# An attention and MLP kernel on one core: less work for first tiles, a split first load, moved weight pieces, and a reordered drain

## The chip, the cores and the metric

The kernel runs on one core of a Trainium2 chip. The metric is the device time of the program in microseconds (us), lower is better. The kernel before took 481.90, 483.58 and 482.17 us in three runs; the median is 482.17.

The engines of a core: TensorE (PE, matrix products, with its weight loads listed apart as PEld), VectorE (DVE), ScalarE (ACT), GpSimd (POOL), and SyncE (SP), which here only issues transfers (DMA). Each works through its own list of instructions; they wait for each other by semaphores.

## The reference

Three layers in a row, in 32-bit floats: an attention with a distance bias and a mask, an MLP mixer, and a gated MLP with a spatial mix. Only the first and the start of the second matter here.

```python
# q, k, v: batch 2, heads 8, seq 768, head_dim 64; n_global = 8, n_local = 96
scores = (q @ k.T) / sqrt(D)
rel = pos[:, None] - pos[None, :]
is_global = pos[None, :] < n_global
is_local = (rel >= 0) & (rel < n_local)
keep = is_global | is_local
dist = where(is_global & ~is_local, n_local, abs(rel))
scores = where(keep, scores - slope[h] * dist, -1e9)
a = softmax(scores)
x = a @ v                          # heads side by side: (2, 768, 512)
h = relu(x.T @ w_tok1) @ w_tok2    # token mix, over the 768 tokens
u = x + h.T
x2 = u + relu(u @ w_ch1) @ w_ch2
# then: u, v = relu(x2 @ w_in) in halves; layer norm of v; spatial mix; gate; w_out
```

## The kernel before

**Tiles.** The 768 positions are six tiles of 128. A query tile needs the keys of its own tile, the last 96 of the tile before, and the first 32 (the global ones). So the host lays out, for each head pair and tile, two blocks of 128 keys: the tile's own, and the tile before with the 32 global keys written over its first columns. For tile 0 the two blocks are: the 32 global keys with zeros behind, and the tile's own. The values are laid out alike. Whether `n_global` and `n_local` fit this form is computed on the device (`flag`); if not, a general path runs (`Else` branches), which is not used with these inputs.

**Pairs and batches.** Two heads (64 rows each) make a pair, 2 x 4 = 8 pairs (`PAIRS`). A batch is two tiles of one pair, so 24 batches (`BATCHES`), three per pair (`PER_PAIR`). q, k and v of a pair lie in one of two buffers. Batches 0, 3, 6, ..., 21 hold tile 0.

**A batch.** `scores(j)`, line 1074: for each tile and head, PE multiplies 128 queries by 256 keys, into PSUM. DVE reads the result with the bias added and takes the maximum (line 830), ACT takes the exponent (line 600), PE transposes the four blocks per tile (`transpose_probs`, line 1063), ACT (line 607, first tile) and DVE (line 838, second tile) copy them out, PE multiplies by the values (`values`, line 1101), ACT copies the product (`oT`, line 612), PE turns it back (`turn_o`, line 1063), DVE divides by the sum into `X32` (line 854), and POOL splits that into a high and a low part `Xh`, `Xl` (`split_batch`, lines 523 and 525). Each code matmul in 32-bit floats appears as two instructions in the trace, a transpose as one.

**The order** is written out by hand on each engine. A round j of PE is: transposes of batch j+1, scores of j+3, values of j, turn of j-1. DVE and ACT have orders of their own, two batches apart.

**Before the first scores** DVE builds `dist` (128 x 384: 128 columns for tile 0's first block, 128 for the own tile, 128 for the tile before) from `rel`, waits for `n_words` (the two counts, 16 bytes per partition, first in SP's queue), and multiplies it by the slopes of heads 0 and 1 (line 817); POOL makes the tables of heads 2 to 7 (line 515). Tile 0 reads columns 0 to 255, other tiles 128 to 383. SP loads q of pair 0, v of 0, q, k, v of 1, ten weight pieces of 256 KB, and then, as buffers come free, `load_qk(n)` after the scores of pair n-2 and `load_v(n)` after its values. ACT issues k of pair 0 (line 593).

**Weight pieces.** A piece lands in a staging slot and is split into a high part (copy) and a low part (subtraction), since later products multiply in three terms, high x high, high x low, low x high (`three`, lines 392 to 394). The first ten (`EARLY_END`: six for the token mix, four for `wc2`) are split by POOL before its first `split_batch` (lines 382 and 387).

**After the attention** PE computes four token products (`x.T @ w_tok1`, 18 matmuls of 512 columns each, two per image), ACT and DVE take the results in two parts (`A1`, line 648) after `attention_done`, which DVE signals when all of `X32` is written. Product 0 and 1 need the first image's x, 2 and 3 the second's (`x_lo`).

Of the kernel before, what the change touches and what calls it, by code (L numbers as in the profile page):

```python
# [21 lines left out]
def build(nc, n_both, qp, kp, vp, w_tok1, w_tok2, w_ch1, w_ch2, w_in, w_spatial, b_spatial, w_out, out):  # L22
# [25 lines left out]
    with ctx:  # L48
# [94 lines left out]
        loc = scratch("loc", [P, 2 * P], F32)  # L143
        tmp = scratch("tmp", [P, 2 * P], F32)
        causal = scratch("causal", [P, 2 * P], F32)
        loc0 = scratch("loc0", [P, GK], F32)
# [35 lines left out]
        flag_ready = sem("flag_ready")  # L182
        ident_ready = sem("ident_ready")
        dist_ready = sem("dist_ready")
        bias_ready = sem("bias_ready")
        pe_passed = sem("pe_passed")
        qk_landed = [sem("qk_landed0"), sem("qk_landed1")]
# [111 lines left out]
        EARLY_END = TOK_END + EARLY  # L299
        C2_END = len(pieces)  # L300
# [127 lines left out]
        def _(sp):  # L428
# [10 lines left out]
            sp.dma_start(qT[:, 0, :], qp[0, 0, :, :]).then_inc(qk_landed[0], 16)  # L439
# [14 lines left out]
            with sp.Else():  # L454
                with sp.Fori(0, B) as b:
                    with sp.Fori(0, HP) as hp:
                        for h in range(2):
                            with sp.Fori(0, NT) as t:
# [5 lines left out]
                                for first, t0, t1 in ((P, 0, 1), (0, 1, NT)):  # L464
# [3 lines left out]
                                for blk, t0, t1 in ((1, 0, 1), (0, 1, NT)):  # L468
# [21 lines left out]
        def _(pool):  # L490
# [40 lines left out]
            def first_pieces():  # L531

                for s in range(EARLY_END):
                    split_hi(pool, s)
                    split_lo(pool, s)
            with pool.If(fast):
                first_pieces()
                for j in range(BATCHES):
                    pool.wait_ge(x_written, j + 1)
                    split_batch(j)  # L540
            with pool.Else():
# [6 lines left out]
                first_pieces()  # L548
# [43 lines left out]
        def _(act):  # L592
            act.dma_start(kk[:, 0, :, :], kp[0, 0, :, :, :]).then_inc(qk_landed[0], 16)

            def exps(j, i):
                if i == 0:
                    wait(act, den_ready, 2 * (j - SUMS) + 1)
                for h in range(2):
                    act.wait_ge(scores_read, 4 * j + 2 * i + h + 1)
                    act.activation(prob[:, j % 3, i, h, :], prob[:, j % 3, i, h, :], ACT.Exp,  # L600
# [3 lines left out]
            def copy_probs(j):  # L604
                act.wait_ge(pt_ready, 2 * j + 1)
                wait(act, o_ready, j - 1)
                act.activation(probT[:, j % 2, 0, :], ps[:, PT, :], ACT.Copy).then_inc(pt_copied_act, 1)
# [37 lines left out]
            for n in range(B * TB):  # L645
                b, tb = divmod(n, TB)
                act.wait_ge(a1_ready, n + 1)
                act.activation(A1[0][:, b, tb, :], ps[:, n, :], ACT.Relu).then_inc(a1_hi, 1)
# [128 lines left out]
        def _(dve):  # L777
            done = [0]

            def step(*instructions):  # L780

                done[0] += len(instructions)
                for ins in instructions:
                    ins.then_inc(dve_setup, 1)
                dve.wait_ge(dve_setup, done[0])

            dve.wait_ge(pool_setup, 3)
            step(dve.tensor_copy(rel[:, :], rel_i[:, :]),
                 dve.tensor_copy(col[:, :], col_i[:, :]),
                 dve.memset(dist[:, GK:P], MASKED))  # L790
            step(dve.tensor_scalar(causal[:, :], rel[:, :], 0.0, None, ALU.is_ge))
# [12 lines left out]
            step(dve.scalar_tensor_tensor(out=loc[:, :], in0=rel[:, :], scalar=nl, in1=causal[:, :],  # L804
                                          op0=ALU.is_lt, op1=ALU.mult),
                 dve.tensor_scalar(glob[:, :], col[:, :], ng, None, ALU.is_lt))
            step(dve.scalar_tensor_tensor(out=loc0[:, :], in0=loc[:, 0:GK], scalar=0.0, in1=glob[:, :],
                                          op0=ALU.is_le, op1=ALU.mult),
                 dve.tensor_scalar(tmp[:, :], loc[:, :], -MASKED, MASKED, ALU.mult, ALU.add),
                 dve.tensor_scalar(glob[:, :], glob[:, :], -MASKED, MASKED, ALU.mult, ALU.add))  # L810
            step(dve.tensor_scalar(loc0[:, :], loc0[:, :], -MASKED, MASKED, ALU.mult, ALU.add),
                 dve.tensor_tensor(dist[:, P:2 * P], rel[:, 0:P], tmp[:, 0:P], ALU.max),
                 dve.tensor_tensor(dist[:, 2 * P + GK:3 * P], rel[:, P + GK:2 * P], tmp[:, P + GK:2 * P], ALU.max),
                 dve.tensor_scalar(dist[:, 2 * P:2 * P + GK], glob[:, :], nl, None, ALU.max))
            step(dve.tensor_scalar(dist[:, 0:GK], loc0[:, :], nl, None, ALU.max))
            dve.sem_inc(dist_ready, 1)
            step(*[dve.tensor_scalar(bias[:, h, :], dist[:, :], -(2.0 ** (-8.0 * (h + 1) / H)) / SCALE, None, ALU.mult)
                   for h in range(2)])

            def scores(j, i):  # L820
# [5 lines left out]
                if t == 0 and b == 0 and hp > 0 and i == 0:  # L826
                    dve.wait_ge(bias_ready, 2 * hp)
                at = 0 if t + i == 0 else P
                for h in range(2):
                    dve.tensor_tensor_reduce(prob[:, j % 3, i, h, :],  # L830
                                             ps[:, SC + 2 * (j % 2) + h, i * 2 * P:(i + 1) * 2 * P],
                                             bias[:, 2 * hp + h, at:at + 2 * P], -SCALE, 3.0e38, ALU.add, ALU.min,
# [26 lines left out]
            scores(0, 0)  # L859
            scores(0, 1)  # L860
# [200 lines left out]
        def _(pe):  # L1061
# [3 lines left out]
            def scores(j):  # L1065

                n, buf, t, b, hp = place(j)
                if t == 0:
# [266 lines left out]
```

## Time and profile before

| | |
|---|---|
| three runs | 481.90, 482.17, 483.58 us |
| profiled execution, its own time | 483.63 us |
| its span (first to last instruction) | 481.8 us |
| PE busy | 469.0 us, 97% |
| DVE, ACT, POOL busy | 187.4, 160.3, 130.2 us |
| DMA moved | 33.10 MB, mean 69 GB/s |

The span is one execution recorded by the hardware profiler; 1.8 us of the time lie outside it. The page gives busy time per engine, the span in forty slices, and the chain that ended last: followed back from the last instruction, at each step to what released it or to the instruction before it on its engine. The other views list instructions in order of time, or sum them over stretches. Matmuls overlap one another, so that a merged piece of several is shorter than their durations summed.

### The profile page before, as it was taken

How to read it: one execution, taken by the hardware profiler on the slowest of the kernel's cores; microseconds unless marked ns; L12 is line 12 of the kernel's file. 1: busy time of each engine (PE TensorE's matmuls, PEld its weight loads, DVE VectorE, ACT ScalarE, POOL GpSimd, SP SyncE). 2: the span in 40 equal slices, each digit the busy share in tenths (PEclk: the TensorE clock that was granted, in tenths of full speed). 3: DMA queues.
4: the chain of work that ended last, by engine and by line, in shares of the span. 5: the costliest groups of instructions: out<-in, count | busy, mean ns of one | idle time of the engine just before them, and what ended most of it. 6: DMA issues, size and time to landing. Idle time of an engine off the chain costs nothing.

```text
span 481.8 us, 7048 instructions
## 1 busy us (share of the span) xinstructions
PE 469.0 (97%) x2664; PEld 400.3 (83%) x2664; DVE 187.4 (39%) x519; ACT 160.3 (33%) x415; POOL 130.2 (27%) x145
## 2 busy tenths in 40 slices
PE   4999999999999999999999999999989999999997
PEld 3777778789988888888888888888879898899985
DVE  5888999426432111511113311104773054204230
ACT  3888888327410000210011211213432213411211
POOL 5996332424232222310002222231670002400000
PEclk9999999999999999999999999999989999999999
DMA  8956545024411121000000011021000100100002
GB/s 323 321 205 236 216 167 199 3 67 152 132 65 45 44 51 60 0 1 0 1 0 0 2 33 34 0 87 35 0 1 0 54 13 1 44 23 1 1 37 94
DMA packets 13618, 33.10 MB, mean 69 GB/s; under 512 B 1552, under 2 KB 3088, under 8 KB 13584
## 3 DMA queue, kind: packets, MB, share of 16 engines
q1 hardware_dynamic: 13440, 31.86, 19.0%
q10 hardware_dynamic: 144, 0.79, 0.4%
q8 instruction: 21, 0.34, 0.3%
q14 instruction: 13, 0.11, 0.1%
HBM read 29.49 MB, written 3.15 MB: 68 GB/s over the span
## 4 chain that ended last, share of the span: by engine, by line
PE 93%; DVE 3%; ACT 1%; DMA 1%; issue 1%; SPq 0%; DVEq 0%
PE ps L392 25%; PE ps L394 25%; PE ps L393 25%; PE ps L1063 6%; PE ps L1074 5%; PE ps L1101 5%; PE ps L1162 1%; DMA qT<-in_q_pairs 1%; DVE V L1021 1%; DVE stats L1012 1%; ACT V L688 1%; DVE xsum L985 0%; DVE wo_h L382 0%; ACT Vn_h L703 0%; DVE xsum L988 0%
## 5 line engine op out<-in xcount | busy, mean ns | idle before, releaser
L997 DVE SCALAR_TENSOR_TENSOR R_l<-ps,R_h 128x512 fp32r<-128x512 f32 x36 | 24.9, 692 | 134.9 <-ACT R_h L674 134.9
L674 ACT ACTIVATE R_h<-ps 128x512 fp32r<-128x512 f32 x36 | 21.4, 595 | 130.5 <-PE ps L394 130.5
L394 PE MATMUL ps<-UT_h,wc_l 128*128 128x512 f32 x144 | 56.0, 389 | 0.0
L393 PE MATMUL ps<-UT_l,wc_h 128*128 128x512 f32 x144 | 56.0, 389 | 0.0
L392 PE MATMUL ps<-UT_h,wc_h 128*128 128x512 f32 x144 | 56.0, 389 | 0.0
L600 ACT ACTIVATE prob<-prob,neg_max 128x256 f32<-128x256 f32 x96 | 47.5, 498 | 7.3 <-DVE neg_max L830 7.3
L567 POOL TENSOR_TENSOR UT_l<-xsum,UT_h 128x512 fp32r<-128x512 f32 x12 | 16.3, 1365 | 84.3 <-ACT UT_h L665 84.3
L392 PE MATMUL ps<-R_h,wc2a 128*128 128x512 f32 x96 | 37.3, 389 | 0.0
L393 PE MATMUL ps<-R_l,wc2a 128*128 128x512 f32 x96 | 37.3, 389 | 0.0
L394 PE MATMUL ps<-R_h,wc2a 128*128 128x512 f32 x96 | 37.3, 389 | 0.0
L830 DVE CUSTOM_DVE_ANT_0 prob<-ps,bias 128x256 f32<-128x256 f32 x96 | 35.6, 412 | 0.7 <-PE ps L1074 0.7
L1074 PE MATMUL ps<-kk,qT 64*128 64x256 f32 x192 | 28.8, 423 | 6.4 <-DMA qT<-in_q_pairs 6.4
L392 PE MATMUL ps<-wsp_h,Vn_h 128*128 128x384 f32 x96 | 32.8, 342 | 2.2 <-DVE xsum L985 2.2
L393 PE MATMUL ps<-wsp_l,Vn_h 128*128 128x384 f32 x96 | 32.8, 342 | 0.0
L394 PE MATMUL ps<-wsp_h,Vn_l 128*128 128x384 f32 x96 | 32.7, 341 | 0.0
L394 PEld LDWEIGHTS ps<-UT_h,wc_l 128*128 128x128 f32 x144 | 27.1, 188 | 5.7
L393 PEld LDWEIGHTS ps<-UT_l,wc_h 128*128 128x128 f32 x144 | 27.0, 188 | 5.6
L392 PEld LDWEIGHTS ps<-UT_h,wc_h 128*128 128x128 f32 x144 | 27.0, 188 | 5.5
L573 POOL TENSOR_TENSOR Vn_l<-V,Vn_h 128x512 fp32r<-128x512 f32 x12 | 16.3, 1362 | 56.0 <-ACT Vn_h L703 56.0
L1035 DVE TENSOR_TENSOR gate<-ps,b_all 128x384 f32<-128x384 f32 x16 | 8.9, 558 | 54.9 <-PE ps L394 54.9
L1074 PEld LDWEIGHTS ps<-kk,qT 64*128 64x128 f32 x192 | 17.7, 198 | 11.8 <-DMA qT<-in_q_pairs 6.4
L1101 PEld LDWEIGHTS ps<-probT,vv 128*64 128x64 f32 x384 | 20.5, 136 | 7.6 <-issue 7.3
(132 smaller groups left out, 1013.8 us busy)
## 6 DMA issues: line engine op xcount, KB each, us to landing
vv<-in_v_pairs SPq DMA_DIRECT2D x8, 768.0 KB, 4.5
kk<-in_k_pairs SPq DMA_DIRECT2D x7, 768.0 KB, 7.3
staged<-in_moe_w_ch SPq DMA_DIRECT2D x20, 256.0 KB, 2.7
qT<-in_q_pairs SPq DMA_DIRECT2D x8, 384.0 KB, 5.2
out<-out_sb SPq DMA_DIRECT2D x12, 256.0 KB, 2.0
staged<-in_moe_w_spatial SPq DMA_DIRECT2D x9, 256.0 KB, 2.6
staged<-in_moe_w_in SPq DMA_DIRECT2D x8, 256.0 KB, 2.6
staged<-in_moe_w_tok SPq DMA_DIRECT2D x6, 256.0 KB, 9.8
```

What stands on the lines that cost most here:

```text
L392: pe.matmul(o, a[0], b[0], start=start, stop=False, skip_group_check=True)
L393: pe.matmul(o, a[0], b[1], start=False, stop=False, skip_group_check=True)
L394: return pe.matmul(o, a[1], b[0], start=False, stop=stop, skip_group_check=True)
L567: pool.tensor_tensor(u, xsum[:, i % 2, :], UT[0][:, d, c * CH:(c + 1) * CH].bitcast(F32), ALU.subtract).then_inc(x2_lo, 1)
L573: pool.tensor_tensor(Vn[1][:, t, :], V32[:, n % 3, :], Vn[0][:, t, :].bitcast(F32), ALU.subtract).then_inc(vn_lo, 1)
L600: act.activation(prob[:, j % 3, i, h, :], prob[:, j % 3, i, h, :], ACT.Exp, bias=neg_max[:, j % 3, i, h:h + 1], scale=-1.0, accum_out=sums ...
L674: act.activation(R[0][:, f % 3, :], ps[:, 4 + f % 4, :], ACT.Relu).then_inc(ring_hi, 1)
L830: dve.tensor_tensor_reduce(prob[:, j % 3, i, h, :], ps[:, SC + 2 * (j % 2) + h, i * 2 * P:(i + 1) * 2 * P], bias[:, 2 * hp + h, at:at + 2 ...
L997: dve.scalar_tensor_tensor(out=R[1][:, f % 3, :], in0=ps[:, 4 + f % 4, :], scalar=0.0, in1=R[0][:, f % 3, :].bitcast(F32), op0=ALU.max, op ...
L1063: return pe.transpose(o, x, ident[:, :])
L1074: last = pe.matmul(ps[:, SC + 2 * (j % 2) + h, i * 2 * P:(i + 1) * 2 * P], qT[rows, buf, (t + i) * P:(t + i + 1) * P], kk[rows, buf, t + i ...
L1101: last = pe.matmul(ps[Dh * h:Dh * (h + 1), OB, o:o + P], vv[:, buf, t + i, blk, h, :], probT[:, j % 2, i, (2 * h + blk) * P:(2 * h + blk + ...
```

## The change

1. *Merged table for first tiles.* Tile 0 uses one key block, its own tile, with a table that takes for the first 32 columns the smaller of the local and the global distance. Its scores, transposes, copies and values are one block wide instead of two (`blocks(j, i)`); other tiles keep two. The host layout follows. DVE's table code has a new order: the 128 columns of tile 0 and their two heads first, the rest (`other_tiles`) after the first reads.
2. *First q, k transfer in two.* The columns for batch 0 come first, counted by `qk_first`; `scores(0)` waits for them, `scores(1)` for the rest.
3. *Weight pieces behind later pairs.* SP issues two pieces after each `load_v(n)`, n = 2 to 6, instead of all ten at the start; POOL splits each between batches.
4. *Tile of ones on PE.* DVE first fills `oT` with ones; PE multiplies it by itself twice (512 columns) into a bank not yet in use, before `scores(0)`.
5. *Token product in the drain.* `token_hidden(0)` is issued before the last turn instead of after it.

The core of the diff:

```diff
+            first = BATCH * P
+            sp.dma_start(qT[:, 0, 0:first], qp[0, 0, :, 0:first]).then_inc(qk_first, 16)
+            sp.dma_start(qT[:, 0, first:S], qp[0, 0, :, first:S]).then_inc(qk_landed[0], 16)
             load_v(0)
             load_qk(1)
             load_v(1)
-            for s in range(EARLY_END):
-                load_piece(sp, s)
...
                     load_qk(n)
                     sp.wait_ge(o_ready, PER_PAIR * (n - 1))
                     load_v(n)
+                    for s in range(2 * (n - 2), min(2 * (n - 1), EARLY_END)):
+                        load_piece(sp, s)
...
+            piece_after = {PER_PAIR * (s // 2) + 2 + s % 2: s for s in range(EARLY_END)}
             with pool.If(fast):
-                first_pieces()
                 for j in range(BATCHES):
                     pool.wait_ge(x_written, j + 1)
                     split_batch(j)
+                    if j in piece_after:
+                        split_piece(piece_after[j])
...
-            act.dma_start(kk[:, 0, :, :], kp[0, 0, :, :, :]).then_inc(qk_landed[0], 16)
+            act.dma_start(kk[:, 0, 0:BATCH, :], kp[0, 0, :, 0:BATCH, :]).then_inc(qk_first, 16)
+            act.dma_start(kk[:, 0, BATCH:NT, :], kp[0, 0, :, BATCH:NT, :]).then_inc(qk_landed[0], 16)
...
+            dve.memset(oT[:, :, :], 1.0).then_inc(ones_ready, 1)
             dve.wait_ge(pool_setup, 3)
...
+            step(dve.tensor_scalar(late[:, 0:P], rel[:, 0:P], nl, MASKED, ALU.is_ge, ALU.mult),
+                 dve.tensor_scalar(glob[:, :], col[:, :], ng, MASKED, ALU.is_ge, ALU.mult))
+            step(dve.tensor_tensor(dist[:, 0:P], rel[:, 0:P], late[:, 0:P], ALU.max),
+                 dve.tensor_scalar(glob[:, :], glob[:, :], nl, None, ALU.max))
+            step(dve.tensor_tensor(dist[:, 0:GK], dist[:, 0:GK], glob[:, :], ALU.min))
+            step(*first_heads(slice(0, P)))
+            step(dve.tensor_scalar(late[:, P + GK:2 * P], rel[:, P + GK:2 * P], nl, MASKED, ALU.is_ge, ALU.mult),
+                 dve.tensor_tensor(dist[:, P:2 * P], rel[:, 0:P], late[:, 0:P], ALU.max),
+                 dve.tensor_copy(dist[:, 2 * P:2 * P + GK], glob[:, :]))
+            def other_tiles():
+                step(dve.tensor_tensor(dist[:, 2 * P + GK:3 * P], rel[:, P + GK:2 * P], late[:, P + GK:2 * P], ALU.max))
+                dve.sem_inc(dist_ready, 1)
+                step(*first_heads(slice(P, 3 * P)))
...
             scores(0, 0)
+            other_tiles()
             scores(0, 1)
...
+        def blocks(j, i):
+            return 1 if j % PER_PAIR == 0 and i == 0 else 2
...
-                        last = pe.matmul(ps[:, SC + 2 * (j % 2) + h, i * 2 * P:(i + 1) * 2 * P],
+                        wide = blocks(j, i) * P
+                        last = pe.matmul(ps[:, SC + 2 * (j % 2) + h, i * 2 * P:i * 2 * P + wide],
                                          qT[rows, buf, (t + i) * P:(t + i + 1) * P],
-                                         kk[rows, buf, t + i, :], start=True, stop=True)
+                                         kk[rows, buf, t + i, 0:wide], start=True, stop=True)
...
+            pe.wait_ge(ones_ready, 1)
+            for _ in range(2):
+                pe.matmul(ps[:, XB, :], oT[:, 0, 0:P], oT[:, :, :].rearrange("p a b -> p (a b)"), start=True, stop=True)
             scores(0)
             scores(1)
...
+                token_hidden(0)
                 turn_o(BATCHES - 1)
...
-            for n in range(B * TB):
+            for n in range(1, B * TB):
+                token_hidden(n)
```

Transposes, copies, exponents and values take `blocks(j, i)` in the same way. `token_hidden(n)` is the body of the former loop.

## Rows read from the trace of the kernel before

**Rows 1.** The page, busy time: engine, us, share of the span, instructions.
```profile
PE 469.0 (97%) x2664; PEld 400.3 (83%) x2664; DVE 187.4 (39%) x519; ACT 160.3 (33%) x415; POOL 130.2 (27%) x145
```

**Rows 2.** The chain in order of time: start us, us, what.
```profile
6.44 3.79 PE ps L1074 x16
10.23 1.98 PE ps L1063 x8
...
14.88 1.06 PE ps L1074 x8
...
84.61 1.02 PE ps L1101 x16
```

**Rows 3.** Timeline of PE, a steady round: start us, us, instruction, count.
```profile
50.27 1.04 PE L1063 MATMUL ps<-ident,prob 128*128 128x128 f32 x8
51.23 1.14 PE L1074 MATMUL ps<-kk,qT 64*128 64x256 f32 x8
52.30 1.09 PE L1101 MATMUL ps<-probT,vv 128*64 128x128 f32 x16
53.32 0.44 PE L1063 MATMUL ps<-ident,oT 128*128 128x128 f32 x2
```

**Rows 4.** Timelines of PE, pieces cut by a window's edge.
```profile
23.84 0.82 PE L1063 MATMUL ps<-ident,prob 128*128 128x128 f32 x6
...
54.56 0.70 PE L1074 MATMUL ps<-kk,qT 64*128 64x256 f32 x4
...
82.76 0.61 PE L1101 MATMUL ps<-probT,vv 128*64 128x128 f32 x8
```

**Rows 5.** Windows, PEld: stretch, us, busy (instructions), clock, DMA share, GB/s.
```profile
51.33:51.44 0.11, 0.11 (x4) 1.00 0.00 0
```

**Rows 6.** Windows, one round: busy of PE, PEld, DVE, ACT, POOL.
```profile
50.27:53.60 3.33, 3.33 (x37) 2.61 (x36) 3.06 (x12) 2.82 (x11) 1.13 (x2) 1.00 0.00 0
```

**Rows 7.** Timeline, the same round, DVE after its wait; idle before in brackets.
```profile
50.53 0.42 DVE L854 TENSOR_TENSOR X<-ps,recip 128x256 f32<-128x256 f32 x1 [0.27 <-PE ps L1063]
```

**Rows 8.** Timeline of the start: DVE to the first read, and a POOL split.
```profile
5.02 0.17 DVE L796 CAST n_lo<-n_words 128x2 f32<-128x2 uint32 x1 [2.67 <-DMA n_words<-in_n_both]
...
5.62 0.48 DVE L804 SCALAR_TENSOR_TENSOR loc<-rel,n_val,causal 128x256 f32<-128x256 f32 x1 [0.17 <-DVE n_val L798]
...
7.93 0.94 DVE L817 TENSOR_SCALAR bias<-dist 128x384 f32<-128x384 f32 x2
8.90 0.42 DVE L830 CUSTOM_DVE_ANT_0 prob<-ps,bias 128x256 f32<-128x256 f32 x1
...
16.09 1.28 POOL L387 TENSOR_TENSOR wt_l<-staged,wt_h 128x512 fp32r<-128x512 f32 x1 [0.15 <-POOL wt_h L382]
```

**Rows 9.** DMA queues from 3.0 to 3.75 us (q10 ACT's, q1 SP's).
```profile
DMA packets 94, 0.29 MB, mean 386 GB/s; under 512 B 47, under 2 KB 47, under 8 KB 94
...
q10 hardware_dynamic: 47, 0.29, 92.4%
```

**Rows 10.** DMA issues from 53 to 56 us, and the windows after them.
```profile
kk<-in_k_pairs SPq DMA_DIRECT2D x1, 768.0 KB, 7.3
...
54.40:59.40 5.00, 5.00 (x53) 3.75 (x52) 4.73 (x18) 4.49 (x16) 2.20 (x4) 1.00 0.98 354
```

**Rows 11.** Timeline of the attention's end.
```profile
89.41 0.44 PE L1063 MATMUL ps<-ident,oT 128*128 128x128 f32 x2
...
90.53 0.41 PE L1063 MATMUL ps<-ident,oT 128*128 128x128 f32 x2 [0.68 <-DVE X L854]
...
90.91 0.47 PE L392 MATMUL ps<-Xh,wt_h 128*128 128x512 f32 x1
...
95.34 0.60 ACT L648 ACTIVATE A_h<-ps 128x512 fp32r<-128x512 f32 x1 [5.43 <-PE ps L394]
```

**Rows 12.** Timeline and windows near 353 us: PE after its idle, clock 0.50.
```profile
352.85 0.41 PE L392 MATMUL ps<-wsp_h,Vn_h 128*128 128x384 f32 x1 [2.19 <-DVE xsum L985]
...
353.60:356.90 3.30, 3.30 (x13) 3.30 (x12) 1.73 (x3) 1.64 (x3) 3.30 (x3) 0.50 0.02 5
```

More of the change, by code:

```diff
@@ L453, in _ @@
                     load_v(n)
+                    for s in range(2 * (n - 2), min(2 * (n - 1), EARLY_END)):
+                        load_piece(sp, s)
             with sp.Else():
+                for s in range(EARLY_END):
+                    load_piece(sp, s)
                 with sp.Fori(0, B) as b:
@@ L529, in _, with split_piece @@
             fast = pool.value_load(flag[0:1, 0:1], min_val=0, max_val=1)
[L531 to L535, printed above, removed]
+            def split_piece(s):
+                split_hi(pool, s)
+                split_lo(pool, s)
+            piece_after = {PER_PAIR * (s // 2) + 2 + s % 2: s for s in range(EARLY_END)}
             with pool.If(fast):
[L537 removed]
                 for j in range(BATCHES):
@@ L547, in _ @@
                 pool.iota(a_col_i[:, :], pattern=[[1, S]], base=0, channel_multiplier=0).then_inc(pool_setup, 1)
-                first_pieces()
+                for s in range(EARLY_END):
+                    split_piece(s)
                 pool.wait_ge(a_x, UNITS * 2 + 1)
@@ L785, in step @@
                 dve.wait_ge(dve_setup, done[0])
+            dve.memset(oT[:, :, :], 1.0).then_inc(ones_ready, 1)
             dve.wait_ge(pool_setup, 3)
             step(dve.tensor_copy(rel[:, :], rel_i[:, :]),
-                 dve.tensor_copy(col[:, :], col_i[:, :]),
-                 dve.memset(dist[:, GK:P], MASKED))
-            step(dve.tensor_scalar(causal[:, :], rel[:, :], 0.0, None, ALU.is_ge))
+                 dve.tensor_copy(col[:, :], col_i[:, :]))
+            step(dve.tensor_scalar(late[:, :], rel[:, :], 0.0, MASKED, ALU.is_lt, ALU.mult))
+            step(dve.tensor_tensor(rel[:, :], rel[:, :], late[:, :], ALU.max))
             dve.wait_ge(n_landed, 16)
@@ L811, in _ @@
[L811 to L816, printed above, removed]
@@ new lines, in _, with first_heads @@
+            step(dve.tensor_tensor(dist[:, 0:GK], dist[:, 0:GK], glob[:, :], ALU.min))
+            def first_heads(columns):
+                return [dve.tensor_scalar(bias[:, h, columns], dist[:, columns], -(2.0 ** (-8.0 * (h + 1) / H)) / SCALE,
+                                          None, ALU.mult) for h in range(2)]
+            step(*first_heads(slice(0, P)))
+            step(dve.tensor_scalar(late[:, P + GK:2 * P], rel[:, P + GK:2 * P], nl, MASKED, ALU.is_ge, ALU.mult),
+                 dve.tensor_tensor(dist[:, P:2 * P], rel[:, 0:P], late[:, 0:P], ALU.max),
+                 dve.tensor_copy(dist[:, 2 * P:2 * P + GK], glob[:, :]))
@@ L1112, in turn_o, with token_hidden @@
                 last.then_inc(xb_ready, 1)
+            pe.wait_ge(ones_ready, 1)
+            for _ in range(2):
+                pe.matmul(ps[:, XB, :], oT[:, 0, 0:P], oT[:, :, :].rearrange("p a b -> p (a b)"), start=True, stop=True)
             scores(0)
             scores(1)
+            def token_hidden(n):
+                b, tb = divmod(n, TB)
+                if n == 0:
+                    wait_pieces(pe, 0, TOK_END)
+                if tb == 0:
+                    pe.wait_ge(x_lo, BATCHES // B * (b + 1))
+                for t in range(NT):
+                    last = three(pe, ps[:, n, :], [w[:, t, tb * P:(tb + 1) * P] for w in wt1],
+                                 [x[:, b * NT + t, :] for x in (Xh, Xl)], t == 0, t == NT - 1)
+                last.then_inc(a1_ready, 1)
             pe.wait_ge(ident_ready, 1)
@@ L1144, in _ @@
                     last.then_inc(a_o, 1)
-            wait_pieces(pe, 0, TOK_END)
-            for n in range(B * TB):
-                b, tb = divmod(n, TB)
-                if tb == 0:
-                    pe.wait_ge(x_lo, BATCHES // B * (b + 1))
-                for t in range(NT):
-                    last = three(pe, ps[:, n, :], [w[:, t, tb * P:(tb + 1) * P] for w in wt1],
-                                 [x[:, b * NT + t, :] for x in (Xh, Xl)], t == 0, t == NT - 1)
-                last.then_inc(a1_ready, 1)
+                token_hidden(0)
+            for n in range(1, B * TB):
+                token_hidden(n)
             for n in range(B * DB * 2):
```

58 lines of the change are left out of this document (27 added, 31 removed).

## The prediction

> **What bounds the kernel now.** I read the page first: TensorE (PE) is busy 97% of the span [rows 1]. The edits lie in the first 91 us, so the chain in order of time comes next [rows 2]. Until 6.44 us PE waits for the first q and k. From there to 14.88 us the chain hops between PE, VectorE (DVE) and ScalarE (ACT): a ramp. From 14.88 to 84.61 us PE alone is on it. The timeline of PE shows a round of that stretch: eight transposes, eight score matmuls, sixteen value matmuls, two turns, from 50.27 to 53.60, no idle time on a row [rows 3]. In that round DVE is busy 3.06 us of 3.33 and ACT 2.82 [rows 6]; DVE would be the next bound. The end of the attention shows a PE wait before the last turn [rows 11]. Ahead of the attention DVE builds the bias table [rows 8].
>
> I sum against the profiled execution's own time, 483.63 us (span 481.8, 1.8 around it). The timed runs were 481.90, 482.17 and 483.58, so the profiled one is like the slowest. Its extra 1.5 us has a visible source: for 3.3 us from 353.6 the granted clock is 0.50, that is 1.2 GHz of 2.4, after PE had idled 2.19 us [rows 12]. Half of 3.3 us is 1.65. I take it that the median run lacks this.
>
> **One key block for first tiles.** Batches that begin with tile 0 (8 of 24, one per head pair) use one block there.
> Transposes: 2 of 8 go. A piece with six lasts 0.82 us, one with eight 1.04 [rows 3, 4]: 0.11 each, so 0.22.
> Values: 4 of 16 go. The two heads run as a pair; x8 against x16 is 0.61 against 1.09 us [rows 3, 4], 0.12 a pair of instructions. I take 0.11, as for a transpose, which also streams 128 columns: 0.22.
> Scores: 4 of 8 instructions shrink from 256 to 128 columns. x4 against x8 is 0.70 against 1.14, 0.21 to 0.22 per pair of heads [rows 3, 4]. If a narrow pair costs the 0.11 of 128 columns, two save 0.21. Bounds: 0, if loading 128 columns of weights for each head is the limit, and 0.21. I take 0.21, because between 51.33 and 51.44 four weight loads of this line were under way [rows 5]: the heads load side by side, a pair per 0.11 us.
> The Trainium skill (TensorE: Matmul & The Clock Gate, LDWEIGHTS) says that a load takes its columns, 107 ns for 128, whatever the rows. Taken one after the other, a narrow pair would stay at 0.21 and the sum would be 1.5 us smaller; taken side by side it agrees with the row.
> The steady stretch holds scores and transposes of seven pairs (pair 0's are in the ramp) and values of eight: 7 x 0.22 + 8 x 0.22 + 7 x 0.21 = **4.8 us**. Is it all on the path? Three rounds fall from 9.99 to 9.34 us on PE. DVE needs 3 x 3.06 = 9.18, less two reads shortened from 256 to 128 columns (0.42 us each now [rows 8], some 0.13 less): 8.9. ACT needs 8.5 less narrower work. PE stays the bound by 0.4 us in three rounds. The shortest PE round is 3.33 - 0.43 = 2.90, 0.16 below DVE's 3.06, and DVE is early by 0.27 us a round, which it spends waiting for PE's turn [rows 7].
>
> **The start.** Four edits, one question: when are the first scores read, now at 8.90 [rows 8], and what follows?
> DVE's path. It takes up n_words at 5.02, starts the first wide operation 0.60 later and reads 3.28 after that [rows 8]. New order before the first read: compares of 128 and 32 columns, then max of each, 0.45 a step; min of 32, 0.25; two heads of 128, 0.45 (two of 384 took 0.94); then compare of 160, max of 128, copy of 32, 0.7. Together 2.3 us: DVE saves 1.0.
> n_words. 16 bytes per partition, yet DVE idled 2.67 us for it [rows 8]. In 0.75 us both queues moved 47 packets: every small one takes turns with a 6 KB one of k [rows 9]. The first k transfer now has 2 KB packets, a third of the time: 47 packets in 0.75 us on 16 engines are 0.25 us each, so the five to six turns still ahead of each engine at 3.0 us shrink from 1.4 us to 0.5. Bounds for the gain 0 and 1.0; I take 1.0, as the turns are seen one to one.
> The Trainium skill (DMA: Bandwidth & Descriptors, Queues, rings and completion order) lets an engine drain some 9 to 17 descriptors of one queue before it turns to the other. Then k's packet size would hardly matter to n_words and the gain would be 1.0 us smaller. The row disagrees.
> So DVE could read at 8.90 - 2.0 = 6.9.
> PE's path. The first scores need 128 KB of q and 256 KB of k. Q comes behind n_words and alternates with the rest of k, so 0.9 of the former 1.15 MB pass first; at the 386 GB/s of [rows 9] 0.7 us sooner, 5.75 instead of 6.44. Sixteen score instructions took 3.79 us [rows 2], 0.47 a pair; this batch has two wide and two narrow pairs, 1.4 us and 0.2 for the last to end: 7.4. At twice the clock it is 6.6.
> The product of ones is four instructions of 512 columns, 0.85 us each by that slow pace (0.43 to 0.47 for 256), from about 1.5 us, behind a memset on DVE, which waits for POOL then anyway, to 5.0. It ends before q arrives. Before, transposes at 10.23 took 1.98 us for eight [rows 2] against 1.04 later [rows 3]: the slow level lasted until about 12. From 1.5 on, the same 6 us would raise the clock about the first scores. If the ones do nothing for the clock, S(0) and S(1) still end by 9.3, before their readers come to S(1).
> First read between 6.9 and 7.9; I take 7.2, 1.7 sooner.
> After it. The other tiles' table (a max, two heads of 256 columns: 1.0 us) now stands before the second pair of reads. From first read to the steady scores at 14.88 it took 6.0 us. Add 1.0, less 0.3 for two narrow reads, less 0.5 for transposes at full clock: 6.2. Steady scores start at 13.4: **1.5 us**, bounds 0.6 and 2.1. POOL's tables for the other heads start, as now, near 8 and are needed two at a time from batch 3 on.
>
> **Weight pieces later.** Ten pieces of 256 KB leave the start, where nothing waited for them: 0. Now two follow the v of pairs 2 to 6 on SP's queue, ahead of the next pair's q and k. K issued at 54.27 landed 7.3 us later, at 61.6; 512 KB more at 354 GB/s add 1.5, and two more issues lie under the transfer: 63.1. That pair's scores are due at 64.56, 63.9 with shorter rounds [rows 10]. Cover 0.8 us; cost 0. POOL splits a piece in 1.28 us and a cast [rows 8], beside 1.13 of its own per round [rows 6]: it fits, and no one waits for it before 83 us.
>
> **Token product in the drain.** Turn 22 starts at 89.41, turn 23 at 90.53 after 0.68 us idle, token matmuls at 90.91 [rows 11]. With 18 token matmuls before turn 23 the idle time goes: **0.7 us**; bounds 0.5 and 0.8. They need the first image's x alone. Later by some 4 us come the last x, attention_done and POOL's split of it; they are wanted by product 2, a whole product after turn 23 (product 0 started at 90.91 and ACT took its result at 95.34 [rows 11]), and take some 2. ACT's first copy waits for attention_done about as long as for its product now.
>
> **Sum.** 4.8 + 1.5 + 0.7 = 7.0 us: 483.63 becomes 476.6 with the slow stretch, 482.17 becomes **475.2** for the median.
>
> **Rivals.**
> A, narrow scores save nothing (weights loaded one after the other), 1.5 back: 476.7. For it: both heads load as many columns as before; against it [rows 5]. Chance 0.17.
> B, the slow clock stretch is in the median run: two of four executions have the longer time, and the edits shift the work. The Trainium skill (the same TensorE page, HAM oscillation) has the clock fall after idle PE. From [rows 12]: plus 1.6, 476.8. Chance 0.17.
> C, n_words lands as before and the ones do nothing: first read 7.9, gain of the start 0.8, 475.9. Chance 0.1.
> D, slower: pieces hold up q and k. It decides once k lands over 0.8 us behind my 63.1. At half the rate (3 us for two pieces) and with both issues unhidden (0.7) it lands at 65.3, 1.4 us late; five pairs cost 7.0 and eat the gain, and a little slower still ends at 483 to 484. Against: the rate in the row. Chance 0.03.
> E, no change to speak of: a chain through DVE, not PE, paces the rounds at 3.33; only start and drain remain, 480.0. Against: DVE's wait in [rows 7]. Chance 0.05.
> The forecast has 0.48. The range goes down by the start's upper bound (0.6), the drain's (0.1) and as much again for what neither bound holds, to 473.8, and up just past A and B, 477.7. This measurement tells about 0.5%, 2.4 us, from no change: faster 0.91, within 0.06, slower 0.03.
>
> **What would show it.** Ones on PE from about 1.5 us; n_lo near 4.0; first read near 7.2; steady scores at 13.4; three rounds in 9.3 us; narrow score pieces 0.2 shorter; no PE wait for q or k at a pair change; no idle time before the last turn, and token matmuls from 83.5. I am wrong if rounds stay at 3.33, if PE waits for DMA at batches 9, 12, 15, 18 or 21, or if the first read stays above 8 us.

## The result and the profile after

The changed kernel takes 475.62 us in the median of four runs (475.02, 475.26, 475.98, 476.14), the kernel before 482.03 (now four runs). The ratio of the means is 0.9856, 95% interval 0.9837 to 0.9875: 6.9 us (6.0 to 7.9) faster; the medians alone differ by 6.4. The profiled execution took 476.14 us with a span of 474.1, against 483.63 and 481.8: 7.5 us in its own time, 7.7 in the span.

I cut both traces at four instants: the start of batch 3's scores, the start of the last value matmuls, the first matmul of token product 1 (the second of the four products), and ACT's first copy (`UT_h`) of what follows the token mix. What lies behind the last is the same in both, 372.9 us. All the gain is ahead of it:

| stretch | before, us | after, us | gain |
|---|---|---|---|
| to the scores of batch 3 | 14.81 | 12.66 | 2.15 |
| from there to the last values | 73.58 | 69.07 | 4.51 |
| from there to token product 1 | 6.69 | 5.56 | 1.13 |
| from there to ACT's first copy of `UT_h` | 13.83 | 13.95 | -0.12 |

The timeline of PE in the kernel after, the start. Columns as in [rows 3], with the idle time before in brackets:

```profile
1.45 3.78 PE L1142 MATMUL ps<-oT 128*128 128x512 f32 x4 [1.45 <-DVE oT L802]
5.16 2.23 PE L1099 MATMUL ps<-kk,qT 64*128 64x128 f32 x16
7.39 0.53 PE L1085 MATMUL ps<-ident,prob 128*128 128x128 f32 x2
9.11 0.93 PE L1085 MATMUL ps<-ident,prob 128*128 128x128 f32 x4 [1.19 <-ACT prob L612]
...
12.66 0.93 PE L1099 MATMUL ps<-kk,qT 64*128 64x128 f32 x8
```

The ones run from 1.45; the first scores come at 5.16 (6.44 in [rows 2]) and sixteen take 2.23 us instead of 3.79. Part of that is less work, since eight of the sixteen are half as wide. The rest is the clock: without the ones the same sixteen take 3.47 us (below). The timeline of all engines shows what DVE does meanwhile, to be held against [rows 8]:

```profile
3.46 0.17 DVE L812 CAST n_lo<-n_words 128x2 f32<-128x2 uint32 x1 [0.76 <-DMA n_words<-in_n_both]
...
6.32 0.29 DVE L851 CUSTOM_DVE_ANT_0 prob<-ps,bias 128x128 f32<-128x128 f32 x1
...
7.15 0.80 DVE L827 TENSOR_SCALAR bias<-dist 128x256 f32<-128x256 f32 x2
7.99 0.42 DVE L851 CUSTOM_DVE_ANT_0 prob<-ps,bias 128x256 f32<-128x256 f32 x1
```

n_words came 1.56 us sooner, the first read 2.58. The chain that ended last (start us, us, what) says who holds the second pair of reads:

```profile
0.74 2.63 DMA n_words<-in_n_both
...
5.24 0.40 DVE bias L827 x2
...
7.15 0.81 DVE bias L827 x2
...
10.08 0.69 DVE probT L859
```

From the landing of n_words to 8.41 every piece but "issue" is DVE's.

A steady group of three rounds, PE's timeline and then the windows (columns as in [rows 6]):

```profile
21.80 0.93 PE L1099 MATMUL ps<-kk,qT 64*128 64x128 f32 x8
22.65 0.88 PE L1127 MATMUL ps<-probT,vv 128*64 128x128 f32 x12
...
27.07 0.82 PE L1085 MATMUL ps<-ident,prob 128*128 128x128 f32 x6
...
78.98 1.25 PE L1085 MATMUL ps<-ident,prob 128*128 128x128 f32 x8
```

```profile
21.80:31.15 9.35, 9.35 (x98) 7.25 (x97) 8.91 (x39) 8.04 (x31) 7.01 (x11) 1.00 0.75 266
```

Scores of a batch with tile 0 last 0.93 instead of 1.14 ([rows 3]), values 0.88 instead of 1.09, transposes 0.82 instead of 1.04. Three rounds take 9.35 us, PE busy throughout, DVE 8.91. The last line of the timeline is the one exception: the transposes of batch 23 take 1.25 us. The second half of their weight loads waits 0.23 us for DVE's copy of the batch before, which ends at 79.51; ACT's last exponent ends at 79.50, so either would hold them:

```profile
78.83 0.68 DVE L859 COPY probT<-ps 128x512 f32<-128x512 f32 x1
79.00 0.50 ACT L612 ACTIVATE prob<-prob,neg_max 128x256 f32<-128x256 f32 x1
79.56 0.42 PEld L1085 LDWEIGHTS ps<-ident,prob 128*128 128x128 f32 x4 [0.23 <-DVE probT L859]
```

The end of the attention, to be held against [rows 11]:

```profile
82.76 0.44 PE L1085 MATMUL ps<-ident,oT 128*128 128x128 f32 x2
82.95 0.48 PE L392 MATMUL ps<-Xh,wt_h 128*128 128x512 f32 x1
...
87.15 0.38 PE L1085 MATMUL ps<-ident,oT 128*128 128x128 f32 x2
87.29 0.47 PE L392 MATMUL ps<-Xh,wt_h 128*128 128x512 f32 x1
```

No idle time stands on these rows; the last turn is two matmuls between two products.

### The profile page after: what moved, and what is told of

Its sections match the earlier page's. It is cut to its first block, busy times and chain, and to the rows that moved or that the text cites. A ratio compares the mean times of both kernels' runs of the same rounds, so it can differ in the third digit from the quotient of the medians.

```text
span 474.1 us, 6965 instructions
## 1 busy us (share of the span) xinstructions
PE 465.6 (98%) x2620; PEld 395.1 (83%) x2620; DVE 186.5 (39%) x521; ACT 156.9 (33%) x415; POOL 129.7 (27%) x145
## 4 chain that ended last, share of the span: by engine, by line
PE 92%; DVE 4%; ACT 2%; issue 1%; DMA 1%; ACTq 0%; DVEq 0%
PE ps L392 25%; PE ps L394 25%; PE ps L393 25%; PE ps L1085 6%; PE ps L1127 5%; PE ps L1099 4%; PE ps L1198 1%; DVE V L1043 1%; DVE stats L1034 1%; ACT V L703 1%; DMA n_words<-in_n_both 1%; DVE xsum L1007 0%; DVE wo_h L382 0%; ACT Vn_h L718 0%; ACT prob L612 0%
## 5 line engine op out<-in xcount | busy, mean ns | idle before, releaser
L612 ACT ACTIVATE prob<-prob,neg_max 128x256 f32<-128x256 f32 (+1 forms) x96 | 45.8, 480 | 4.8 <-DVE neg_max L851 4.6
L851 DVE CUSTOM_DVE_ANT_0 prob<-ps,bias 128x256 f32<-128x256 f32 (+1 forms) x96 | 33.6, 389 | 0.9 <-PE ps L1099 0.5
L1085 PE MATMUL ps<-ident,prob 128*128 128x128 f32 x176 | 24.4, 275 | 1.4 <-ACT prob L612 1.4
L1099 PE MATMUL ps<-kk,qT 64*128 64x256 f32 (+1 forms) x192 | 25.6, 385 | 0.1
L1127 PEld LDWEIGHTS ps<-probT,vv 128*64 128x64 f32 x352 | 18.7, 136 | 7.7 <-issue 7.3
```

Of the source, the lines that this page charges most:

```text
L612: act.activation(p, p, ACT.Exp, bias=neg_max[:, j % 3, i, h:h + 1], scale=-1.0, accum_out=sums[:, j % SUMS, i, h:h + 1]).then_inc(probs_re ...
L851: dve.tensor_tensor_reduce(prob[:, j % 3, i, h, 0:wide], ps[:, SC + 2 * (j % 2) + h, i * 2 * P:i * 2 * P + wide], bias[:, 2 * hp + h, at:a ...
L1085: return pe.transpose(o, x, ident[:, :])
L1099: last = pe.matmul(ps[:, SC + 2 * (j % 2) + h, i * 2 * P:i * 2 * P + wide], qT[rows, buf, (t + i) * P:(t + i + 1) * P], kk[rows, buf, t + ...
L1127: last = pe.matmul(ps[Dh * h:Dh * (h + 1), OB, o:o + P], vv[:, buf, t + i, blk, h, :], probT[:, j % 2, i, c:c + P], start=blk == 0, stop=b ...
```

## The experiments

All but one start from the changed kernel; diffs are against it, shortened at `...`, and a comment on a line may stand for more of the same edit. Each trace was cut at the same instants; "stretch" is that from batch 3's scores to the last values. Seven of the edits were timed in one execution only; for them the trace counts, not the time.

**Wide scores**

```diff
-                        wide = blocks(j, i) * P
+                        wide = 2 * P      # scores on PE only
```

> The changed kernel, with the scores of a first tile computed 256 columns wide again (the second half is not read). In the changed kernel it is 69.07 us from the start of the scores of batch 3 (12.66) to the start of the last values (81.73). Theory: a narrow pair of heads costs 0.11 us against 0.21, so seven batches give back 7 x 0.21 = 1.5 us: 70.5 us for that stretch, and 1.5 us in the time. Rival A: narrow scores save nothing, the stretch stays at 69.1. Rival E (a chain through DVE paces the rounds): also 69.1, since DVE's work is the same.

Measured: stretch 70.53 us, 1.46 more than 69.07. Median 478.55, ratio to before 0.9907 (0.9871 to 0.9943): by the ratios 2.5 us slower than the changed kernel where 1.5 was expected, with intervals of 0.9 and 1.7 us either way, so the times alone don't decide, the stretch does. The theory holds; PE, not a chain through DVE, paces the rounds, and the heads' weight loads don't hold a narrow pair.

**Transposes and values of first tiles added back**

```diff
+                            if blocks(j, i) == 1:
+                                last = tr(ps[:, PT + i, c + 2 * P:c + 3 * P], prob[:, j % 3, i, h, 0:P])
...
+                    if blocks(j, i) == 1:
+                        for h in range(2):     # the same product again
+                            last = pe.matmul(..., start=True, stop=True)
```

> The changed kernel, with the two transposes and four value matmuls per first tile added back on PE as repeats (same result, DVE and ACT unchanged). Theory (PE paces the rounds): 7 x 0.22 + 8 x 0.22 = 3.3 us back, the stretch from scores of batch 3 to the last values 69.1 to 72.4 us; at most 0.2 less where the end of the attention waits for ACT. Rival E: it stays under 70.

Measured: 72.12 us, 3.05 more; median 478.95, ratio 0.9919 (0.9893 to 0.9945). It lacks 0.25 of 3.3, the 0.2 at the end among it: with the longer values of batch 21 back, the transposes of batch 23 no longer wait. The two experiments add up to 1.46 + 3.05 = 4.51 us, the whole gain of the stretch.

**No ones**

```diff
-            dve.memset(oT[:, :, :], 1.0).then_inc(ones_ready, 1)
...
-            pe.wait_ge(ones_ready, 1)
-            for _ in range(2):
-                pe.matmul(ps[:, XB, :], oT[:, 0, 0:P], ...)
```

> The changed kernel without the memset of ones and the product of ones. Theory: the granted clock then rises some 6 us after the first scores at 5.2, near 11 us, as in the kernel before (12.2); but DVE, not PE, leads to the first read (6.32) and the second (7.99), so it loses only where slow scores or transposes are late: first read after 5.2 + 1.6 = 6.8 instead of 6.3, transposes slower, scores of batch 3 at about 13.4 instead of 12.66. Rival (ones do nothing): 12.7. Rival (ones are the larger part of the start's gain): over 14.

Measured: first read 6.83, scores of batch 3 at 13.16, time 476.69. Its timeline of PE, to be held against that of the changed kernel above:

```profile
5.01 3.47 PE L1098 MATMUL ps<-kk,qT 64*128 64x128 f32 x16 [5.01 <-DMA qT<-in_q_pairs]
8.41 0.44 PE L1084 MATMUL ps<-ident,prob 128*128 128x128 f32 x2
```

The scores are slow (3.47 us for sixteen), as expected, but the transposes after 8.4 are fast already, sooner than I thought. And 13.16 is no clear loss: seven executions with the ones and an unchanged n_words had that instant at 12.55, 12.66, 12.88, 12.94, 12.99, 13.25 and 13.41. What the ones are worth here can't be told from nothing: 0.6 us by the earliest of these, less than nothing by the latest. All eight have one thing in common: batch 3's scores start 6.33 or 6.34 us after the first read. So the spread arises before that read, which lies between 6.21 and 7.08 in the seven and at 6.83 here.

**k of pair 0 in one transfer**

```diff
-            act.dma_start(kk[:, 0, 0:BATCH, :], kp[0, 0, :, 0:BATCH, :]).then_inc(qk_first, 16)
-            act.dma_start(kk[:, 0, BATCH:NT, :], kp[0, 0, :, BATCH:NT, :]).then_inc(qk_landed[0], 16)
+            act.dma_start(kk[:, 0, :, :], kp[0, 0, :, :, :]).then_inc(qk_first, 16)
+            act.sem_inc(qk_landed[0], 16)
```

> The changed kernel with k of pair 0 as one transfer with packets of 6 KB again (q stays split). Theory (each small packet of n_words takes turns with one packet of k): n_words reaches DVE near 5.0 us instead of 3.46, first read near 7.9 instead of 6.32, scores of batch 3 near 14.2 instead of 12.66. Rival (the Trainium skill's page DMA: Bandwidth & Descriptors, an engine drains a packet of many descriptors before it turns to the other queue): n_words stays near 3.5, and only the first scores of PE come later, 5.9 instead of 5.2: scores of batch 3 at 12.7 to 13.3.

Measured: n_words at DVE 4.96, first read 7.77, scores of batch 3 at 14.11, time 477.68. The DMA view from 3.0 to 3.75 us of this kernel, then from 2.25 to 3.0 of the changed one (packets, MB, share of 16 engines; q1 is SP's queue, with n_words):

```profile
q10 hardware_dynamic: 45, 0.28, 92.5%
q1 hardware_dynamic: 45, 0.00, 3.3%
```

```profile
q10 hardware_dynamic: 101, 0.19, 75.4%
q1 hardware_dynamic: 98, 0.02, 18.1%
```

Turns one to one in both, twice as many with small packets. The rule of the Trainium skill (DMA: Bandwidth & Descriptors, Queues, rings and completion order), by which an engine drains many descriptors before it changes queues, does not describe these runs: n_words is 128 packets, eight per engine if they are shared evenly, which one such drain would take at once, and yet 45 of them still move here between 3.0 and 3.75 us. The size of k's packets moved n_words by 1.5 us, and with it all that follows by 1.45.

**Pieces at the start**

```diff
             load_v(1)
+            for s in range(EARLY_END):
+                load_piece(sp, s)
...
-                    for s in range(2 * (n - 2), min(2 * (n - 1), EARLY_END)):
-                        load_piece(sp, s)
```

with POOL's splits ahead of its batches again.

> The changed kernel with all ten weight pieces back at the start (SP's queue, and POOL's splits before the batches). Theory: moving them was worth 0: scores of batch 3 at 12.7, stretch to the last values 69.1, both within 0.1. Rival (pieces crowded the loads of pair 1 or 2, or POOL's backlog held something): PE waits for q and k at batch 3 or 6, up to 1 us later.

Measured: stretch 71.63 us, 2.56 longer. PE's timeline and the DMA issues between 11 and 16 us, here and in the changed kernel (the last column of a DMA line is us from issue to landing):

```profile
24.69 0.93 PE L1097 MATMUL ps<-kk,qT 64*128 64x128 f32 x8 [2.50 <-DMA kk<-in_k_pairs]
```

```profile
kk<-in_k_pairs SPq DMA_DIRECT2D x1, 768.0 KB, 10.5
```

```profile
kk<-in_k_pairs SPq DMA_DIRECT2D x1, 768.0 KB, 6.2
```

My theory fell, and the rival was too mild. k of pair 2, issued at 14.19, stood behind the pieces and landed 10.5 us later; batch 6's scores waited 2.50 us for it. In the changed kernel it is issued at 11.52 and lands 6.2 us later. In the kernel before, with the pieces at the start, the same k was issued at 14.34:

```profile
kk<-in_k_pairs SPq DMA_DIRECT2D x1, 768.0 KB, 9.8
```

So it landed at about 24.1, for scores at 24.58: a cover of 0.4 us, which the faster start uses up.

**All pieces behind q and k of pair 2**

```diff
                     load_qk(n)
+                    if n == 2:
+                        for s in range(EARLY_END):
+                            load_piece(sp, s)
```

> The changed kernel with all ten weight pieces in one run on SP's queue, but behind q and k of pair 2 instead of ahead of them (with the pieces at the start PE waited 2.50 us for that k at batch 6, 24.69). Theory (k of pair 2 landed late because it stood behind 2.5 MB of pieces in the one queue): no wait at batch 6; stretch from scores of batch 3 to the last values 69.1 again. Rival (the bytes themselves crowd the transfers, wherever they stand): a wait of 1 us or more at batch 6 or 9.

Measured: no wait on PE for a transfer from 12.5 us to the last values, stretch 69.06, scores of batch 6 at about 22.4; 475.13 us. So it is the place in the queue, not the bytes.

**Four pieces per pair**

```diff
-                    for s in range(2 * (n - 2), min(2 * (n - 1), EARLY_END)):
+                    for s in range(4 * (n - 2), min(4 * (n - 1), EARLY_END)):
```

with POOL's splits after batches 3 to 12.

> The changed kernel with four weight pieces per pair behind v of pairs 2 and 3, and two behind pair 4, instead of two behind pairs 2 to 6. Two pieces add 1.5 us to the landing of the next k, four 3.0. Theory (cover 0.8 us over two pieces): PE waits for q or k about 0.7 us at batches 9 and 12, 1.4 us in all. Rival D, milder (cover already gone at two): PE would wait over 1.5 us twice. Rival (cover is larger than computed): no wait at all.

Measured: batch 9's scores start 0.2 us late, at 32.10, stretch 69.27, time 475.58. That is far less than the 1.4 us expected, but not because two pieces alone leave more cover than 0.8 us. The changed kernel's own issues say what they leave. k of pair 3, from the timeline and the DMA view:

```profile
22.63 0.57 SPq L436 DMA_DIRECT2D kk<-in_k_pairs  x1
```

```profile
kk<-in_k_pairs SPq DMA_DIRECT2D x1, 768.0 KB, 8.1
```

It lands at 30.73 for scores at 31.15: a cover of 0.4 us. Read in the same way, k of pairs 4 to 7 lands 1.6, 0.7, 0.7 and 0.6 us ahead. Over six traces with two pieces per pair and the same rounds (the changed kernel, the runs without ones, with k in one transfer and with the turn first, and the two better starts below), pair 4 has 1.5 to 1.7 us each time, pair 3 anything from 0.4 to 1.6. With four pieces the k of pair 4, issued at 34.22, lands 7.2 us later, at 41.42, for scores at 41.45. So two more pieces cost 1.6 us there, near the 1.5 priced, and just use up that cover. The k of pair 3, issued at 24.59, lands at 32.09, and its scores are the late ones. In the changed kernel the 0.8 us that I had computed is about right for pairs 5 to 7, and here these got no more than two pieces.

**Last turn first again**

```diff
-                token_hidden(0)
                 turn_o(BATCHES - 1)
+                token_hidden(0)
```

> The changed kernel with the last turn before token product 0 again. From the turn of batch 22 to the first matmul of token product 1 it is 4.53 us in the changed kernel and 5.67 in the kernel before. Theory: 5.67 again here, 1.1 us lost. Rival (the prediction's size): only 0.7 lost, the rest of the 1.14 belonging to something else: 5.2.

Measured: 5.50 us from turn 22 to token product 1, 477.04 us.

```profile
82.97 0.44 PE L1085 MATMUL ps<-ident,oT 128*128 128x128 f32 x2
84.09 0.41 PE L1085 MATMUL ps<-ident,oT 128*128 128x128 f32 x2 [0.68 <-DVE X L875]
84.26 0.48 PE L392 MATMUL ps<-Xh,wt_h 128*128 128x512 f32 x1
```

The idle 0.68 us are back, 0.97 us in all. The other 0.17 of 1.14 is not the order: from the last turn to the first token matmul it takes 0.17 us here and took 0.38 in [rows 11], where the product stood behind the end of the `If`; here it stands inside. That this place is the cause was not tried alone.

**The merged table alone**

```diff
-            dve.memset(oT[:, :, :], 1.0).then_inc(ones_ready, 1)     # and the product of ones
-            sp.dma_start(qT[:, 0, 0:first], qp[0, 0, :, 0:first]).then_inc(qk_first, 16)
-            sp.dma_start(qT[:, 0, first:S], qp[0, 0, :, first:S]).then_inc(qk_landed[0], 16)
+            sp.dma_start(qT[:, 0, :], qp[0, 0, :, :]).then_inc(qk_first, 16)
...
+            act.dma_start(kk[:, 0, :, :], kp[0, 0, :, :, :]).then_inc(qk_first, 16)
...
                 turn_o(BATCHES - 1)
+                token_hidden(0)
```

and the pieces at the start again.

> Of the five edits only the merged table and single block with DVE's new order stay; ones, split loads, moved pieces and moved token product are undone. Theory, from the terms: n_words at 5.0, first read near 8.3 (DVE's chain alone saves 0.6 to 1.0, and slow scores end near 8.2), scores of batch 3 near 14.3; stretch 69.1; drain as before. Time before minus 0.5 minus 4.5, about 477. Rival (edits overlap): under 476.

Measured: stretch 69.07 as expected, but first read 8.20 and scores of batch 3 only at 15.73, 1.4 us later than expected and later than the 14.81 of the kernel before; median 480.09 where about 477 was expected, ratio 0.9943 (0.9921 to 0.9966). Its timeline of PE:

```profile
6.37 3.36 PE L1096 MATMUL ps<-kk,qT 64*128 64x128 f32 x16 [6.37 <-DMA qT<-in_q_pairs]
...
10.99 1.18 PE L1082 MATMUL ps<-ident,prob 128*128 128x128 f32 x4 [0.63 <-ACT prob L610]
12.10 2.08 PE L1096 MATMUL ps<-kk,qT 64*128 64x256 f32 x8
14.11 1.69 PE L1082 MATMUL ps<-ident,prob 128*128 128x128 f32 x8
```

Eight wide scores take 2.08 us where 1.13 is the pace at the full clock: here the clock stayed low until about 15 us. From the first read to batch 3's scores it takes 7.5 us instead of 6.3. PE is idle between its short pieces in the ramp (0.63 us before one of them), and the clock rose 9 us after its first matmul, against 3.3 in the kernel without ones and 5.8 in the kernel before. (The clock column of the windows shows 1.00 until the first change on record; before that the pace of the matmuls tells the level.) The pieces stand at the start here too, and nothing waits for k of pair 2: issued at 14.63, it lands 9.8 us later, at 24.43, for scores at 24.86.

**The kernel before with the ones alone**, against the kernel before:

```diff
+            dve.memset(oT[:, :, :], 1.0).then_inc(ones_ready, 1)
...
+            pe.wait_ge(ones_ready, 1)
+            for _ in range(2):
+                pe.matmul(ps[:, XB, :], oT[:, 0, 0:P], oT[:, :, :].rearrange("p a b -> p (a b)"), start=True, stop=True)
             scores(0)
```

> The kernel before with the memset and the product of ones alone. Theory: the clock rises near 5.5 us instead of 12.2, so the first scores and transposes run fast; the first read is held by DVE's table (8.87 at the earliest), so it stays near 8.9, and scores of batch 3 start 0.5 to 1.0 us sooner, about 14.0 instead of 14.81; then k of pair 2, landed 9.8 us after its issue at 14.34 and due at 24.58, has no cover left: PE waits up to 0.5 us for it at batch 6. Rival (ones do nothing without the other edits): 14.8 and no wait.

Measured: first read 8.89, scores of batch 3 at 15.32, 0.5 us later than without ones; no wait for k; 482.80 us beside 481.90 for the kernel before. The timeline and two windows of PE (stretch, us, busy, clock):

```profile
6.37 2.00 PE L1076 MATMUL ps<-kk,qT 64*128 64x256 f32 x16 [1.54 <-DMA qT<-in_q_pairs]
10.01 2.16 PE L1065 MATMUL ps<-ident,prob 128*128 128x128 f32 x8 [1.65 <-ACT prob L601]
12.10 2.08 PE L1076 MATMUL ps<-kk,qT 64*128 64x256 f32 x8
```

```profile
8.40:10.00 1.60, 0.00 (x0) 1.00 1.03 430
11.20:14.40 3.20, 3.20 (x14) 0.50 1.04 363
```

The theory was half right: the first sixteen scores ran at the full clock (2.00 us instead of 3.79). But their readers were no sooner, so PE, which had idled 1.54 us before those scores, idled 1.65 us behind them; the granted clock fell to 0.50 (1.2 GHz) at 11.1, and the work that does lie on the path, transposes and scores from 10 to 14.4, ran slow.

**A better start: ACT makes half of the first table**

```diff
+            act.wait_ge(dist_first, 1)
+            second_head(slice(0, P))       # activation Copy with head 1's slope as its scale
+            act.wait_ge(dist_ready, 1)
+            second_head(slice(P, 3 * P))
             exps(0, 0)
...
-            step(*first_heads(slice(0, P)))        # DVE: two heads
+            dve.sem_inc(dist_first, 1)             # DVE: head 0 alone, in the next step
```

and the last step of `dist` moved ahead of the first read.

> The changed kernel, with ACT, idle until the first exponent at 6.66, computing head 1's part of the bias table while DVE computes head 0's, and the distance for other tiles finished before the first read. DVE then has 0.6 us less before its second pair of reads. Theory (the chain of the start runs through DVE from n_words to the reads at 7.99): second reads at about 7.3, scores of batch 3 at about 12.0 instead of 12.66, time 0.6 us less. Rival (ACT's tables delay its first exponents, and these lead): scores of batch 3 at 12.6 or later.

Measured: second reads at 7.24, scores of batch 3 at 11.91, median 473.69 us of five runs, ratio to before 0.9819 (0.9792 to 0.9845). The changed kernel's was 0.9856 (0.9837 to 0.9875), timed on another occasion; the intervals overlap, so between the two kernels the times alone are no proof. In the traces the start is shorter: 11.91 against 12.55 to 13.41 in the seven named above, and the stretch is the same 69.07.

**The same with token product 0 in three parts**

```diff
+                    if j == BATCHES - 2:
+                        token_hidden(0, 0, 1)
+                    if j == BATCHES - 1:
+                        token_hidden(0, 1, 2)
...
-                token_hidden(0)
+                token_hidden(0, 2, NT)
```

> The kernel with ACT's table, and in the drain token product 0 in pieces: 3 of its 18 matmuls before the transposes of batch 23, 3 before the last values, 12 before the last turn. Theory: PE's waits for ACT there (0.2 us in the transposes, 0.35 of weight loads before the last values) are filled, 0.3 us less than with ACT's table alone. Rival: each switch to the product costs about 0.15 us, and nothing is gained.

Measured: 473.55 us, ratio 0.9818 (0.9792 to 0.9845). From batch 3's scores to token product 1 it takes 74.49 us against 74.64, only 0.15 us less. The theory holds all the same: from batch 21's scores to token product 1 it takes 18.39 us against 18.75, so the drain gains 0.36. But 0.2 is lost at batch 15, whose k, issued at 40.65, landed at 49.35 for scores due at 49.17, and they started 9.58 us after batch 12's instead of 9.35:

```profile
kk<-in_k_pairs SPq DMA_DIRECT2D x1, 768.0 KB, 8.7
```

```profile
49.40 0.93 PE L1113 MATMUL ps<-kk,qT 64*128 64x128 f32 x8
```

In the kernel without this edit the same k took 7.6 us. Nothing in the edit touches that load, so this looks like the spread of the transfers: two pieces per pair leave a cover that can be gone in a single execution.

## Why the prediction was right, and where it was not

The forecast of 475.2 us is 0.4 below the median of 475.62, inside 473.8 to 477.7. The sum was 7.0 us, the traces show 7.7, the ratio 6.9. Two terms were too small and one too large, so that the closeness is in part luck. The median of the changed kernel lies between two runs with the slow stretch of rival B and two without; the forecast was for runs without it, and these took 475.02 and 475.26.

*Steady stretch, 4.8 forecast, 4.51 measured.* Each of its terms was confirmed by adding it back: scores 1.46 for 1.5, transposes and values 3.05 for 3.3. What lacks is the last pair: PE wins 0.2 us in the values of batch 21 and gives it back in batch 23's transposes, where DVE's copy and ACT's last exponent both end at 79.5. DVE stayed under PE (8.91 of 9.35 us, forecast 8.9 of 9.34), and rivals A and E are refuted.

*Start, 1.5 forecast, 2.15 measured.* The step on n_words was right in kind and too small in size: 1.56 us sooner where I set 1.0, for I counted only the turns after 3.0 us, not those before. Another 0.3 is the margin by which I set the first read at 7.2 and not at the 6.9 that came out of DVE's path; it was not needed. The chain of DVE took 2.86 us from n_lo to the first read, forecast 2.9. After the first read it took 6.34 us, forecast 6.2. But this instant is not a constant: over the seven executions named above it lies between 12.55 and 13.41, by and large later where the clock rises later (5.0 to 6.6 us). The profiled execution is one of the early ones. With the mean of the seven, 12.95, the start is worth 1.9.

*Drain, 0.7 forecast, 1.13 measured.* The idle time of 0.68 us is only part: undoing the order cost 0.97. With the product next, its first matmul starts 0.19 us after turn 22 does and overlaps its end; with turn 23 next, turn 22 takes its whole 0.44 us before the idle time begins. Another 0.17 comes, as far as the traces tell, from the product's place inside the `If`. And 0.12 is given back behind token product 1's start: there it takes 13.95 us in the changed kernel, where the last turn stands right ahead of that product and its second matmul starts 0.32 us after the first, and 13.84 in the run with the turn first again, where this is 0.23.

*Weight pieces, 0 forecast.* This is the step that failed, without harm to the sum. "Nothing waited for them" was read from a trace in which k of pair 2 had 0.4 us left. With the rest of the change in place the pieces at the start cost 2.5 us, so moving them is what lets the start's gain arrive. With the slow start of the merged table alone they cost nothing. The cover behind the moved pieces was well priced: 0.8 us forecast, 0.7 measured for that pair, though 0.4 for the thinnest. Rival D did not come: pieces ahead of later q and k cost nothing in the changed kernel, and four per pair 0.2. But the last experiment lost 0.2 us to a late k with two per pair, so that the margin is thin.

*Ones.* I counted them as harmless, and gave them half a microsecond after the first read. In the changed kernel their worth isn't resolved (at most 0.6 us); in the kernel before they cost 0.5, by one execution of each. Whether they pay hangs on what comes right behind them.

*Rival B* was real and came on both sides. For 3.3 us the clock of the changed kernel's profiled execution is at the lower level too:

```profile
346.70:350.00 3.30, 3.30 (x12) 3.30 (x11) 0.96 (x1) 0.94 (x2) 3.30 (x4) 0.50 0.00 0
```

Behind ACT's first copy of `UT_h` the traces with this stretch take 372.8 to 372.9 us (before, after, and five others), the seven without it 371.3 to 371.4: 1.5 us. What decides it is open: PE idles 2.19 us ahead of the fall here, and 2.16 at the same place of the better start's trace, where no fall follows. Two of the four runs of the changed kernel have it by their mean clock (0.995, 0.996), two do not (1.000).

## What to carry to other kernels

A transfer that nothing waits for in today's trace can be the next wait once something else gets faster: before calling it free, subtract the gain upstream from its slack (here 0.4 us of slack, for scores that came due some 2.4 us sooner). When one engine is busy in every round, count its instructions by the pitch between pieces, check the next engine's busy time per round, and the sum can be trusted to some 6%. A tiny transfer in one queue pays for the packet size of the other queue.

## What the runs showed of the hardware

Two hardware queues took turns packet by packet: 45 against 45, and 101 against 98, in 0.75 us. A warm-up of PE can be lost again: in the kernel before with ones the clock rose at 4.3 us, fell at 11.1 after idle stretches of 1.54 and 1.65 us, and rose at 14.5. From the first matmul to the rise it took 2.9 to 9 us, depending on the kernel and the execution. Two score instructions with 64 rows and 128 columns, one for each head, cost together what one transpose does, 0.11 us. The same 768 KB behind two pieces took 7.0 to 8.1 us from issue to landing within one execution.
